# A chain of conditions at the end of an expert loop: nested instead of in a row

## The reference

```python
expert_idx = np.argmax(x @ w_gate, axis=1)
for e in range(E):                     # E = 8
    mask = expert_idx == e
    h = np.maximum(x[mask] @ w1[e], 0.0)      # 512 -> 1024
    out[mask] = gate_w[mask, None] * (h @ w2[e])   # 1024 -> 512
```

## Time and profile before

| | |
|---|---|
| time, median of 3 runs | 882.8 us (882.39 to 883.36) |
| profiled execution, its own time | 883.8 us |
| profiled execution, span | 880.1 us |
| TensorE busy | 842.7 us (96%) |
| VectorE, ScalarE, GpSimd busy | 385.7, 298.4 and 217.5 us |
| last matmul starts | 860.58 us |
| last operation on GpSimd starts | 862.56 us |

### The profile page before, as it was taken

The page is one execution under the profiler, slowest core; times in us unless marked ns, Lnnn a source line. Parts: engine busy times, 40 slices in busy tenths (PEclk is TensorE's granted clock), DMA queues, the critical chain, the costliest instruction groups (busy, mean ns, idle before and its releaser), DMA issues.

```text
span 880.1 us, 15343 instructions
## 1 busy us (share of the span) xinstructions
PE 842.7 (96%) x4983; PEld 754.3 (86%) x4984; DVE 385.7 (44%) x735; ACT 298.4 (34%) x694; POOL 217.5 (25%) x196
## 2 busy tenths in 40 slices
PE   6988999999999999999999999999999999999981
PEld 6877899999999999999999999997888888888860
DVE  5877732532272245226323622526225645552430
ACT  5767521221312132112213123434224545442510
POOL 5277899102002000200110003144611111111100
PEclk9999999999999999999999999999999999999996
DMA  6887850020002000200200002225343545553100
GB/s 208 251 302 258 310 201 1 1 72 1 1 1 72 1 1 4 70 1 1 72 1 1 1 36 96 99 86 198 121 155 130 217 141 203 191 204 135 39 21 9
DMA packets 38456, 86.20 MB, mean 98 GB/s; under 512 B 4014, under 2 KB 13230, under 8 KB 38000
## 3 DMA queue, kind: packets, MB, share of 16 engines
q1 hardware_dynamic: 33344, 70.79, 23.3%
q0 software_dynamic: 3360, 10.23, 3.2%
q10 hardware_dynamic: 1680, 4.21, 1.5%
HBM read 71.06 MB, written 14.94 MB: 98 GB/s over the span
## 4 chain that ended last, share of the span: by engine, by line
PE 92%; DVE 2%; DMA 1%; ACT 1%; issue 1%; POOL 1%; SPq 0%; POOLq 0%; ACTq 0%; DVEq 0%
PE ps L946 26%; PE ps L948 26%; PE ps L947 26%; PE ps L891 3%; PE ps L911 2%; PE ps L1099 2%; PE ps L887 2%; DMA kt<-kT 1%; PE ps L991 1%; PE ps L899 1%; PE ps L1017 1%; PE ps L988 1%; ACT pr L669 1%; PE ps L1133 0%; PE ps L877 0%
## 5 line engine op out<-in xcount | busy, mean ns | idle before, releaser
L946 PE MATMUL ps<-xn_hi,GV_hi 128*128 128x384 f32 x576 | 198.4, 345 | 0.5 <-ACT pr L669 0.4
L948 PE MATMUL ps<-xn_hi,GV_lo 128*128 128x384 f32 x576 | 193.3, 336 | 0.0
L947 PE MATMUL ps<-xn_lo,GV_hi 128*128 128x384 f32 x576 | 193.2, 335 | 0.0
L1256 DVE TENSOR_TENSOR silu<-sig,ps 128x384 f32<-128x384 f32 x72 | 39.9, 554 | 176.4 <-ACT sig L717 175.9
L946 PEld LDWEIGHTS ps<-xn_hi,GV_hi 128*128 128x128 f32 x576 | 108.3, 188 | 3.1 <-issue 0.5
L947 PEld LDWEIGHTS ps<-xn_lo,GV_hi 128*128 128x128 f32 x576 | 108.4, 188 | 1.9
L948 PEld LDWEIGHTS ps<-xn_hi,GV_lo 128*128 128x128 f32 x576 | 108.1, 188 | 0.0
L723 ACT ACTIVATE h_hi<-ps 128x384 fp32r<-128x384 f32 x72 | 35.4, 491 | 158.8 <-DVE ps L1261 158.8
L948 PE MATMUL ps<-Wo_hi,h_lo 128*128 128x512 f32 x216 | 85.5, 396 | 0.0
L947 PE MATMUL ps<-Wo_lo,h_hi 128*128 128x512 f32 x216 | 85.3, 395 | 0.0
L946 PE MATMUL ps<-Wo_hi,h_hi 128*128 128x512 f32 x216 | 84.3, 390 | 0.3 <-issue 0.3
(11 more groups left out here) (164 smaller groups left out, 1416.0 us busy)
## 6 DMA issues: line engine op xcount, KB each, us to landing
EW_raw<-w SPq DMA_DIRECT2D x32, 1024.0 KB, 7.2
vt<-vW SPq DMA_DIRECT2D x32, 192.0 KB, 5.2
qraw<-qT SPq DMA_DIRECT2D x16, 288.0 KB, 4.3
kt<-kT SPq DMA_DIRECT2D x16, 288.0 KB, 4.3
xT_rows<-xo SPq DMA_DIRECT2D x16, 288.0 KB, 3.4
xc<-xT_rows SPq DMA_DIRECT2D x6, 768.0 KB, 5.8
y_rows<-ysb SPq DMA_DIRECT2D x6, 768.0 KB, 4.1
vt<-vW SPq DMA_DIRECT2D x16, 128.0 KB, 4.2
```

Of the source, the lines that this page charges most:

```text
L946: nc.tensor.matmul(out, a_hi, b_hi, start=start, stop=False)
L947: nc.tensor.matmul(out, a_hi, b_lo, start=False, stop=False)
L948: return nc.tensor.matmul(out, a_lo, b_hi, start=False, stop=stop)
L1256: nc.vector.tensor_tensor(silu[:], sig[f % 2][:], ps[:, G_BANK + f % 2, 0:CH], ALU.mult).then_inc(silu_ready, 1)
```

## The change

The conditions are nested. `last_tiles` now takes the body as a function and calls itself. At `s` it first asks whether exactly `s + 2` tiles are used; if so, the last two tiles are done in one body. Otherwise it asks whether more are used, and everything that follows, tile `s` with `left=2` and all conditions for later tiles, lies inside that condition. On GpSimd the gathers, scatters and waits for landings of the tiles from 18 on are nested in the same way (`last_rows`, `stored`), and the waits for the landings come in reverse order of the tiles, those of tiles 14 to 17 last. What the tiles compute is the same.

```diff
--- before.py
+++ after.py
@@ -314,15 +314,16 @@
         def used_tiles(eng):
             return eng.value_load(start_i[0:1, E:E + 1], min_val=LEAST, max_val=SLOTS)
 
-        def last_tiles(eng, used):
-
+        def last_tiles(eng, used, tile, s=LEAST - 2):
 
             assert (LEAST - 2) % DEEP == 0
-            for s in range(LEAST - 2, SLOTS):
-                for left in (2, 1, 0):
-                    if LEAST <= s + 1 + left <= SLOTS:
-                        with eng.If(used > s + 2 if left == 2 else used == s + 1 + left):
-                            yield s, left
+            with eng.If(used == s + 2):
+                tile(s, 1)
+                tile(s + 1, 0)
+            if s + 2 < SLOTS:
+                with eng.If(used > s + 2):
+                    tile(s, 2)
+                    last_tiles(eng, used, tile, s + 1)
 
         rounded, splits = (w1_rounded, w2_rounded), (w1_split, w2_split)
 
@@ -632,23 +633,32 @@
             pool.wait_ge(ids_ready, 2)
             pool.wait_ge(eid_ready, 2)
             used = used_tiles(pool)
-            for s in range(SLOTS):
+            def stored(s):
+                pool.wait_ge(o_out[s % DEEP], 16 * (s // DEEP + 1))
+
+            for s in range(LEAST):
                 ahead = s + DEEP - 1
                 if DEEP < ahead < LEAST:
                     gather(ahead)
-                elif LEAST <= ahead < SLOTS:
+                elif ahead >= LEAST:
                     with pool.If(used > ahead):
                         gather(ahead)
-                if s < LEAST:
+                scatter(s)
+
+            def last_rows(s):
+
+                with pool.If(used > s):
+                    if s + DEEP - 1 < SLOTS:
+                        with pool.If(used > s + DEEP - 1):
+                            gather(s + DEEP - 1)
                     scatter(s)
-                else:
-                    with pool.If(used > s):
-                        scatter(s)
-            for u in range(DEEP):
-                pool.wait_ge(o_out[u], 16 * ((LEAST - 1 - u) // DEEP + 1))
-            for s in range(LEAST, SLOTS):
-                with pool.If(used > s):
-                    pool.wait_ge(o_out[s % DEEP], 16 * (s // DEEP + 1))
+                    if s + 1 < SLOTS:
+                        last_rows(s + 1)
+                    stored(s)
+
+            last_rows(LEAST)
+            for s in range(LEAST - DEEP, LEAST):
+                stored(s)
 
 
         @blk.scalar
@@ -862,8 +872,7 @@
                 s0 = 2 * pair
                 for u in range(2):
                     slot_tile(s0 + u, u)
-            for s, left in last_tiles(act, used):
-                slot_tile(s, s % 2, left)
+            last_tiles(act, used, lambda s, left: slot_tile(s, s % 2, left))
 
 
         @blk.tensor
@@ -1174,8 +1183,7 @@
             with pe.Fori(1, (LEAST - 2) // DEEP) as group:
                 for v in range(DEEP):
                     slot_tile(DEEP * group + v, v, 16 * (group + (v + 2) // DEEP) + 16)
-            for s, left in last_tiles(pe, used):
-                slot_tile(s, s % DEEP, 16 * ((s + 2) // DEEP) + 16, left)
+            last_tiles(pe, used, lambda s, left: slot_tile(s, s % DEEP, 16 * ((s + 2) // DEEP) + 16, left))
 
 
         @blk.vector
@@ -1515,8 +1523,7 @@
             with dve.Fori(1, (LEAST - 2) // DEEP) as group:
                 for u in range(DEEP):
                     slot_tile(DEEP * group + u, u, 16 * group)
-            for s, left in last_tiles(dve, used):
-                slot_tile(s, s % DEEP, 16 * (s // DEEP), left)
+            last_tiles(dve, used, lambda s, left: slot_tile(s, s % DEEP, 16 * (s // DEEP), left))
 
 
 def kernel(q, k, v, moe_w_gate, moe_w_val, moe_w_out, moe_rms_g, moe2_w_gate, moe2_w1, moe2_w2):
```

## The result

The changed kernel takes 867.1 us (median of 4 runs, 865.9 to 868.5) against 883.0 us before (4 runs, 882.4 to 883.4). The ratio is 0.9827 with a 95% interval of 0.9808 to 0.9847: 15.9 us faster. The prediction had 871.2 us and a range of 867.8 to 874.0. The profiled execution took 868.5 us for a span of 866.8; that is 1.7 us around the span, where the kernel before had 3.7.

What follows compares the result with a forecast made beforehand. TensorE's false conditions, waiting for code loads after the last tile, were taken to set the end. Span 880.1 - 9.9 - 1.4 - 0.3 = 868.5, 11.6 less; time 882.8 - 11.6 = 871.2 us, range 867.8 to 874.0.

Steps and rivals of the forecast that it cites:

- The time around the span: Execution time beyond the span, 883.8 against 880.1 us before; span differences were carried over to the median unchanged.
- The chain at the end (1, 3): Behind tile 20, TensorE's 15 false conditions (24.0 us) become one jump; GpSimd's drain is then last, span 9.9 us less.
- the three readings of the drain: GpSimd's end drain: takes 3.51 us again (chosen), hangs on the scatter (0.3 us different), or falls to 0.17 us.
- Rival A: GpSimd's drain at the end is short, 0.17 us as at the start: time 867.9 us; chance 0.12.
- The gap before tile 19 (2): No body is skipped from tile 18 to 19, so TensorE's idle 1.42 us goes; bounds 0 and -1.42.
- Rival B: TensorE's stall moves to tiles 16 to 18, costing 1.42 us once or 2.8 twice: 872.6 to 874.0 us; chance 0.12.
- GpSimd's own steps (4): Between last landing and GpSimd's drain, closing branches replace seven conditions: -0.3 us, bounds -1.1 and +0.3.
- The clock (6): TensorE's lower clock in tile 20, after the wait for the split, stays: 0, bounds -1.7 and +2.6 us.
- Rival C: TensorE needs several code loads at its end, for the jump and closing branches: 877.7 us; chance 0.06.
- Rival D: TensorE can't jump far ahead behind the last tile but loads code in order to the target: 886.9 us; chance 0.04.
- Rival E: No difference: something unrecorded in the profile lasts as long as TensorE's chain: 882.8 us; chance 0.02.

Runs made afterwards that it cites:

- the two experiments that take the change apart: Against the kernel before: only TensorE's conditions nested, 869.2 us against 881.7; all engines but TensorE nested, 882.4 us, ratio 0.999.
- TensorE alone: Kernel before with only TensorE's conditions nested, the other engines keeping theirs in a row: 869.2 us against 881.7, ratio 0.984.
- landings on SyncE: Changed kernel with the waits for the scatters' landings moved from GpSimd to SyncE, nested the same way: 865.2 us, ratio 0.979 to the kernel before.
- the changed kernel's second one: The changed kernel run once more, unaltered, beside the version with landing waits on SyncE: 867.3 us against 882.4 for the kernel before, ratio 0.983.
- The kernel without the last body: Kernel before with no body on TensorE under the condition for tile 26, the last of 27: 879.4 us against 882.4, ratio 0.997.
- the single guard: Kernel before with one more condition on TensorE around all conditions from tile 21 on: 869.6 us against 881.7, ratio 0.988.

## Why the prediction fell short of the gain

The chain, the gap and GpSimd's drain came out as told; two other terms failed. The time around the span was taken as constant and fell by 2.0 us, and the clock in tile 20 was put at 0 and brought 1.6 us. Either alone would have left the time within the range (871.2 - 2.0 = 869.2, or 871.2 - 1.6 = 869.6); both together give 867.6, below its lower end of 867.8.

Step by step, on the two profiled executions (880.1 and 866.8 us of span, 13.3 less; 11.6 were forecast):

1. **The chain at the end (1, 3).** Forecast -9.9, with GpSimd's drain of 3.51 us as the new last. Measured: TensorE drains at 858.3, within the 858 to 862 that were forecast, by one long condition of 3.9 us. That time holds the rest of a load that was under way, and yet it isn't the two loads (7.4 us) that were allowed for. From the end of GpSimd's drain to the end of the span there are 0.24 us. Right, and the two experiments that take the change apart put the end of the chain on TensorE. Of the three readings of the drain the first was right: its length is the same in all 11 profiles, counted from its own start or from the end of the last scatter's issue, whichever is later. Rival A is out.
2. **The gap before tile 19 (2).** Forecast -1.42. Measured -1.58 from matmul to matmul, of which 0.28 came back before tile 17. Rival B was right about the place and too dear by far: 0.28 us here, 0.40 in two other profiles with the same nesting on TensorE (TensorE alone, landings on SyncE), and 0.01 in the changed kernel's second one.
3. **GpSimd's own steps (4).** From the start of the last scatter to the drain 3.37 instead of 3.85 us, -0.5; forecast -0.3. In the other profiles this distance is 3.37 to 3.45 us with GpSimd nested and 3.63 to 4.75 with its conditions in a row, so the sign is sure and the size isn't.
4. **The clock (6).** Forecast 0 with bounds -1.7 and +2.6; it came out at the lower one, -1.6 (seven matmuls at 0.43 instead of 0.23 us before, and 0.2 at the borders). It can't be put down to the change for certain, since three kernels with the old gap had the full clock too. This step failed: a single profiled execution with the lower clock was taken for the rule ("That wait stays, so I leave it at 0"). The wait did stay, 1.83 us, and the clock was full. The bound of -1.7 was named, but the range didn't take it in beside the rest. Why the clock fell stays open. The 0.49 us with which the 0.63 is compared belongs to the first matmul after the wait; the others at the full clock take 0.39.
5. **The time around the span.** This is the larger term that failed, and it was put at nothing without a reason: I said how the span would shrink and took what lies around it, 3.7 us, as given ("so I take the differences over to the median"). It fell by 2.0 us in the two profiled executions (3.7 to 1.7), and in all runs of which the span is on record it is 3.4 to 4.3 us before and 1.7 to 1.8 after. The kernel without the last body shows that it hangs on where TensorE's program ends. That it was one more wait for a load, on the same engine, fits the load recorded across the end of the span, but isn't shown.

Sum of the measured: -9.9 - 1.3 - 0.5 - 1.6 = -13.3 of span, and -2.0 around it, 15.3 for the two profiled executions. The medians are 15.9 apart; the profiled execution after was the slowest of its four.

Rival C (several loads at the end) is out: TensorE drains right behind its one long condition. Rival D (the code up to the target is loaded in order) is out: the jump skips what before cost seven long conditions, and took 3.9 us. Rival E is out: the time fell.

## What to carry to other kernels

In this kernel a false condition on TensorE cost 0.21 us over a short body and about 2 us over that of a tile. Where bodies are long, nest the conditions so that the case that occurs is followed by a single jump, or put one guard around the rest, which gave nearly the same here. Look for it where the data are complete long before the span ends, in the drains and in the longest branch on each queue. And compare the time of an execution with its span before taking a difference of spans as a difference of times; what lies behind the last instruction moved here by 2.0 us, and may belong to the same mechanism.

## What the runs showed of the hardware

- Conditions on the last tiles, TensorE: 0.07 to 0.08 us not taken, 0.21 to 0.34 taken without a wait, 1.2 to 3.9 us taken with a load of code under way, and 4.8 in one case, the jump of the single guard; on ScalarE and VectorE 0.03 to 0.07.
- One jump forwards over code that took seven loads to walk past cost one wait, 3.3 to 4.8 us in the five profiles that have it.
- The drain of GpSimd at the end takes 3.51 us in all 11 profiles (in one of them counted from the end of the scatter that was still being issued), whether the last transfer has landed when it begins or not; at the start of the program it took 0.17. What it does in that time the records don't say.
- Taking 45 rows of a body that never runs from the end of TensorE's program moved the time around the span from 3.4 to 4.3 us to 1.7 to 1.9, with no change among the recorded instructions. A load of code lies across the end of the span in both kernels.
